# A routed expert loop over 32-token tiles in four column groups, and slot experts in two banks

## The chip, the cores and the metric

One core of a Trainium2 chip runs the whole program. The core has the engines TensorE (PE, with its weight loads PEld), VectorE (DVE), ScalarE (ACT), GpSimd (POOL) and SyncE (SP), and 16 DMA engines. The metric is device time in microseconds (us) of one execution; lower is better. In this program SP issues the plain transfers and POOL the gathers and scatters by row index.

## The reference

Three stages follow one another: a linear attention with decay over 4 x 8 heads, 768 steps and head size 48; a mixture of experts that sends each chosen token to one of 8 experts; and a soft mixture with 8 experts of 4 slots each. All numbers are float32.

```python
N, D, E, F = (3072, 384, 8, 1024)      # tokens, width, experts, hidden width
...
def _moe_ref(x, w_skip, w_gate, w1, w2):
    do_compute = x @ w_skip > 0
    out = x.copy()
    xc = x[do_compute]
    logits = xc @ w_gate
    e_idx = np.argmax(logits, axis=1)
    ...
    for e in range(E):
        mask = e_idx == e
        h = np.maximum(xc[mask] @ w1[e], 0.0)
        y[mask] = gate_w[mask, None] * (h @ w2[e])
    out[do_compute] = xc + y
...
def _moe2_ref(x, phi, w1, w2):
    logits = x @ phi                    # 32 slots, 4 of each expert
    ...
    slot_input = d.T @ x                # d: softmax of logits over the tokens
    for e in range(E):
        slot_out[e] = np.maximum(slot_input[e] @ w1[e], 0.0) @ w2[e]
    return c @ slot_out                 # c: softmax of logits over the slots
```

With these inputs 1514 of the 3072 tokens are sent to an expert: 194, 234, 156, 201, 198, 219, 156 and 156 to the eight.

## The kernel before

The program is one block with an instruction stream written by hand for each engine; semaphores order them, and nothing is reordered by a scheduler. Attention runs over 16 pairs of heads, then the gate, then a sort: DVE and PE work out a list of row numbers (`take_i`, `put_i`) in which each expert's tokens stand together, padded to whole tiles of 128 rows. Two tiles for each of the eight experts make 16 tiles. `tiles_i` holds where each expert's tiles end; every engine loads these numbers into registers and loops to them.

**The routed expert loop.** For a tile, POOL gathers 128 rows from `tokens` in DRAM (L1206), DVE turns them in 16 blocks (L1100, `V.transpose` of 32x96 each), ACT copies the turned rows into `x_t` (L859). PE computes the hidden layer with the weights stationary, 24 products of 128x128 with 128 tokens (L611); ACT applies the ReLU on the way to `h_t` (L856); PE multiplies by `w2` with `h_t` stationary, 8 products of 128x384 (L622). DVE copies the 128x384 result to `ys` (L1105), and POOL scatters it to `results` in DRAM (L1211). A float32 product shows as two PE records. The next tile's rows are gathered and turned while PE works. The weights of expert e + 2 go into the places of expert e (`w1_sb[e % 2]`, `w2_sb[e % 2]`): SP issues both loads when the last result of expert e has landed in DRAM (`load_ffn`, behind `results_stored`), and one matrix of the slot experts behind them.

**Back and slot scores.** SP loads all result rows (L409), DVE adds them to the tokens (L1125), PE turns the new rows (L649) and multiplies them by `phi` (L638). PE runs `idle_products(32)` (L572) while it waits for the rows.

**The slot experts.** Eight experts times two matrices of 1.5 MB. Those of experts 0 to 3 are loaded in the routed loop. The rest wait for places: `e1` of expert 5 goes where the first eight back tiles lay, `e1` of 4 where the next eight lay, and SP issues 4, 5 and 6 together when all 24 back tiles have been added (`x2_ready`). `e1` of 7 and `e2` of 4 and 5 lie in `x_sb` and wait until PE has used it (`slot_parts_full`). PE computes the hidden layers of all eight experts into one PSUM bank (L707, 32 stationary columns, four column groups side by side by `tile_position`, 256 moving columns); then ACT applies one ReLU (L905), PE turns the result (L718), ACT copies it out (L908, L909), and PE runs the eight second layers (L728, four column groups, 384 moving columns).

**Out.** Two small products fold the parts, and PE, ACT, DVE and SP write the 24 output tiles (L745, L920, L1170, L426).

## Time and profile before

| what | us |
|---|---|
| median of 3 runs (433.33 to 436.28) | 434.66 |
| the profiled execution, whole | 430.86 |
| its span on the core | 429.1 |
| PE busy in the span | 390.1 (91%) |
| DVE, ACT, POOL busy | 262.4, 161.9, 103.4 |
| granted PE clock, mean over the span | 0.981 |

The span runs from the first to the last instruction of the core; the whole execution has 1.76 us around it. The profiled execution is 3.8 us faster than the median of the three timed ones. Busy time of PE counts modelled ends of pipelined products, so the time of a stage is read from start to start, not from busy time.

### The profile page before, as it was taken

The page shows a single profiled execution, that of the slowest core. Times are in us where ns is not written, and L with a number is a line of the kernel's source. Part 1 is how long each engine was busy: PE and PEld are TensorE (multiplying, and loading weights), DVE is VectorE, ACT ScalarE, POOL GpSimd, SP SyncE. Part 2 cuts the span into 40 slices and gives each one's busy share as a digit, 9 for nine tenths or more (in the row PEclk, how much of TensorE's full clock was granted, in tenths as well). Part 3 has the DMA queues.
Part 4 walks back from the last instruction along what each step waited for, and adds up shares of the span by engine and source line. Part 5 has one row for each costly group of instructions (what it writes and reads, how often), then busy time and mean ns, then how long its engine had stood idle before and what let it go on. Part 6 is the DMA issues. An engine that isn't in the chain of part 4 may idle for free.

```text
span 429.1 us, 10101 instructions
## 1 busy us (share of the span) xinstructions
PE 390.1 (91%) x3912; PEld 305.5 (71%) x3913; DVE 262.4 (61%) x547; ACT 161.9 (38%) x464; POOL 103.4 (24%) x133
## 2 busy tenths in 40 slices
PE   0799999999999999899999999999999998999861
PEld 0578877777777887777788888888888887855340
DVE  8999999999999346544444444444445354851042
ACT  1567887787678642011111111111111112831031
POOL 2214424443443500312222222222222220020000
PEclk9979999999999999999999999999999998999997
DMA  8957556756779994111485958586767737599929
GB/s 319 388 183 281 217 198 245 249 191 217 256 237 350 397 409 194 38 37 38 171 330 194 324 203 316 216 299 234 279 244 269 259 108 251 215 392 390 373 98 361
DMA packets 40977, 106.97 MB, mean 249 GB/s; under 512 B 3552, under 2 KB 23264, under 8 KB 40432
## 3 DMA queue, kind: packets, MB, share of 16 engines
q1 hardware_dynamic: 38704, 99.62, 62.9%
q0 software_dynamic: 2240, 6.88, 4.7%
q8 instruction: 24, 0.39, 0.4%
q14 instruction: 9, 0.07, 0.1%
HBM read 88.80 MB, written 17.69 MB: 248 GB/s over the span
## 4 chain that ended last, share of the span: by engine, by line
PE 51%; DMA 9%; DVE 6%; issue 1%; ACT 1%; DVEq 0%; POOLq 0%; POOL 0%; ACTq 0%
PE a_bank L611 20%; PE y_bank L622 19%; DMA e_sb<-in_moe_w 4%; DMA x_sb<-in_moe_w 3%; PE a_bank L649 3%; PE a_bank L532 2%; DVE x_sb L1170 1%; PE y_bank L638 1%; DMA results<-ys,put_now 1%; DMA work<-tokens,take_i 1%; DMA back<-results 1%; PE a_bank L669 1%; DVE k_in L955 1%; PE sums_bank L540 1%; ACT bonus_v L790 1%
## 5 line engine op out<-in xcount | busy, mean ns | idle before, releaser
L611 PEld LDWEIGHTS a_bank<-batch_t,w_sb 128*128 128x128 f32 x768 | 88.2, 192 | 5.3 <-issue 1.3
L611 PE MATMUL a_bank<-batch_t,w_sb 128*128 128x128 f32 x768 | 88.4, 275 | 1.1 <-issue 1.1
L1100 DVE STREAM_TRANSPOSE work<-parts 32x96 f32<-32x96 f32 x256 | 69.1, 270 | 28.0 <-DMA parts<-tokens,take_now 24.7
L622 PE MATMUL y_bank<-w_sb,work 128*128 128x384 f32 x256 | 85.2, 486 | 0.0
L1193 POOL TENSOR_SCALAR_AFFINE_SELECT a_sb<-a_sb 128x512 f32<-128x512 f32 x48 | 50.7, 1058 | 86.5 <-ACT a_sb L780 86.5
L622 PEld LDWEIGHTS y_bank<-w_sb,work 128*128 128x128 f32 x256 | 47.4, 190 | 29.7
L856 ACT ACTIVATE work<-a_bank 128x512 f32<-128x512 f32 x32 | 19.1, 597 | 130.8 <-PE a_bank L611 130.8
L1105 DVE COPY ys<-y_bank 128x384 f32<-128x384 f32 x16 | 8.9, 558 | 68.2 <-PE y_bank L622 68.2
L790 ACT ACTIVATE bonus_v<-v_sb,bonus 128x48 f32<-128x48 f32 x192 | 44.9, 327 | 0.0
L469 PE MATMUL a_bank<-r_in,k_in 64*128 64x128 f32 x384 | 36.9, 314 | 1.5 <-DVE r_in L956 0.5
L469 PEld LDWEIGHTS a_bank<-r_in,k_in 64*128 64x128 f32 x384 | 27.2, 200 | 11.7 <-issue 6.7
L933 DVE TENSOR_TENSOR_SCAN decay<-wrk_sb,ones_at 128x780 f32<-128x780 f32 x16 | 28.5, 1778 | 1.2
L942 DVE TENSOR_TENSOR_SCAN decay<-wrk_sb,inv_at 128x780 f32<-128x780 f32 x16 | 28.8, 1802 | 0.1
L780 ACT ACTIVATE a_sb<-a_bank 128x512 f32<-128x512 f32 x48 | 28.5, 593 | 0.6 <-PE a_bank L469 0.6
L490 PE MATMUL y_bank<-r_in,state 64*48 64x128 f32 x320 | 21.4, 276 | 3.9 <-DVE x_sb L969 3.9
L495 PE MATMUL y_bank<-a_sb,v_sb 128*48 128x128 f32 x384 | 24.3, 276 | 0.0
L490 PEld LDWEIGHTS y_bank<-r_in,state 64*48 64x48 f32 x320 | 18.2, 160 | 6.5 <-issue 6.1
L439 PE MATMUL ktok_bank<-ident,k_in 128*128 128x128 f32 x64 | 10.6, 290 | 12.8 <-DVE k_in L955 12.8
L495 PEld LDWEIGHTS y_bank<-a_sb,v_sb 128*48 128x48 f32 x384 | 20.2, 123 | 2.4
L1206 POOL DMA_INDIRECT parts<-tokens,take_now x17 | 18.1, 1064 | 14.6 <-POOL take_now L1236 13.8
L1211 POOL DMA_INDIRECT results<-ys,put_now x17 | 17.8, 1045 | 15.3 <-POOL put_now L1240 14.4
L955 DVE TENSOR_TENSOR k_in<-wrk_sb,decay 128x768 f32<-128x768 f32 x16 | 20.0, 1252 | 0.2 <-PE a_bank L469 0.2
(234 smaller groups left out, 480.9 us busy)
## 6 DMA issues: line engine op xcount, KB each, us to landing
w_sb<-in_moe_w SPq DMA_DIRECT2D x20, 1536.0 KB, 10.7
wrk_sb<-in_wrk SPq DMA_DIRECT2D x16, 768.0 KB, 7.3
e_sb<-in_moe_w SPq DMA_DIRECT2D x8, 1536.0 KB, 14.8
wrk_sb<-in_wrk SPq DMA_DIRECT2D x15, 780.0 KB
v_sb<-in_vt SPq DMA_DIRECT2D x16, 288.0 KB, 2.8
results<-work SPq DMA_DIRECT2D x1, 4608.0 KB, 15.1
tokens<-x_sb SPq DMA_DIRECT2D x4, 1152.0 KB, 14.1
x_sb<-in_moe_w SPq DMA_DIRECT2D x3, 1536.0 KB, 15.4
```

The costliest lines, as they stand in the source:

```text
L469: last = nc.tensor.matmul(a_bank[:, 2 * (g % 2) + a, (c % 2) * C:(c % 2 + 1) * C], k_in[rows, cols], r_in[n % 3][rows, cols], start=True, ...
L490: nc.tensor.matmul(y_cols[64 * a:64 * a + D, c * C:(c + 1) * C], state[n % 2][rows, :, c - 1], r_in[n % 3][rows, c * C:(c + 1) * C], start ...
L495: last = nc.tensor.matmul(y_cols[64 * a:64 * a + D, c * C:(c + 1) * C], v_sb[n % 4][:, c, a, :], a_sb[n % 2][:, a, c, :], start=False, sto ...
L611: last = nc.tensor.matmul(bank[2 + f // 4][:, (f % 4) * P:(f % 4 + 1) * P], w1_sb[j][:, kk, f * P:(f + 1) * P], x_t[:, kk, :], start=(kk = ...
L622: last = nc.tensor.matmul(bank[4][:, 0:DM], h_t[:, f, :], w2_sb[j][:, f, :], start=(f == 0), stop=(f == FK - 1))
L780: nc.scalar.activation(a_sb[n % 2][:, :, 2 * s:2 * s + 2, :].rearrange("p a c t -> p a (c t)"), a_bank[:, 2 * (g % 2):2 * (g % 2) + 2, 0:2 ...
L790: last = nc.scalar.activation(bonus_v[n % 2][:, c, a, :], v_sb[n % 4][:, c, a, :], ACT.Copy, scale=bonus[:, c, a:a + 1])
L933: V.tensor_tensor_scan(decay[:, 0:SCAN], wrk_sb[i][:, 0:SCAN], ones_at[:, :], 0.0, ALU.mult, ALU.add).then_inc(mid_up_ready, 1)
L942: V.tensor_tensor_scan(decay[:, SCAN:2 * SCAN], wrk_sb[i][:, SCAN:2 * SCAN], inv_at[:, :], 0.0, ALU.mult, ALU.add).then_inc(mid_down_ready, 1)
L955: V.tensor_tensor(by_half(k_in[:, :]), by_half(k), half_rows(decay, 0, 3 * NC, True), ALU.mult).then_inc(k_ready, 1)
L1100: last = V.transpose(turned_rows[SQ * o:SQ * (o + 1), :, SQ * i:SQ * (i + 1)], rows_by_block[SQ * i:SQ * (i + 1), :, SQ * o:SQ * (o + 1)])
L1193: nc.gpsimd.affine_select(out=x, in_=x, compare_op=ALU.is_gt, fill=0.0, base=0, pattern=[[0, 2], [0, 2], [1, C]], channel_multiplier=-1).t ...
```

## The change

The routed loop goes over tiles of 32 tokens. Each expert's rows are padded to a multiple of 32 (at least one tile), all of them together to a multiple of 128; the counts above give 7, 8, 5, 7, 7, 7, 5 and 5 tiles, 51, and 52 with the last padding: 13 groups of four. Rows are still gathered and scattered 128 at a time, once for a group.

For a tile the tokens are now stationary (128x32) and the weights move: the hidden layer is 3 x 4 products of 256 columns (`first_layer`), the second 4 x 4 products of 192 columns (`second_layer`), four column groups side by side. PE issues the first layer of a tile before the second layer of the tile ahead of it. DVE turns a group's rows in one instruction (128x384) and the hidden layer in one (128x256); ACT and DVE copy two 32x96 blocks each for a tile's `x_t`; ACT copies two halves of the second layer's result (64x192 each) and DVE adds them in two instructions of 32x192. POOL copies the first 96 rows of a finished group from `ys` to `ys_out`, DVE adds the last 32 there directly. `w2` is laid out in DRAM by partition. SP loads `w1` of expert e + 2 when the last first layer of expert e is done, and `w2` when its last second layer is done. PE runs 42 idle products at the end of the loop in place of 32, and two between the loads of each of the eight loop ends.

`e1` of slot experts 5 and 4 is issued after 8 and 16 added tiles, `e1` of 7 after the first half of the dispatch. The slot experts' hidden layers 0 to 3 and 4 to 7 go to two banks, with a ReLU and a turn for each; the second layers of 0 to 3 start before the second half has been turned.

```diff
...
+            FB = F // PER
+            YW = DM // 2
...
             for e in range(E):
                 j = e % 2
-                over = sp.snap(16 * end + 16)
-                sp.wait_ge(results_stored, over)
-                sp.wait_ge(ld_ffn[j], 32 * (e // 2 + 1))
+                sp.wait_ge(h_full, end)
+                sp.wait_ge(ld_w1[j], 16 * (e // 2 + 1))
                 if e < E - 2:
-                    load_ffn(sp, e + 2)
+                    load_w1(sp, e + 2)
+                sp.wait_ge(ffn_done, end)
+                sp.wait_ge(ld_w2[j], 16 * (e // 2 + 1))
+                if e < E - 2:
+                    load_w2(sp, e + 2)
                     (load_e1, load_e2)[e % 2](sp, e // 2)
...
+            def first_layer(j, x, out):
+
+                for kk in range(DK):
+                    for g in range(PER):
+                        last = nc.tensor.matmul(out[SUB * g:SUB * (g + 1), 0:FB], x[:, kk, :], w1_sb[j][:, kk, FB * g:FB * (g + 1)],
+                                                start=(kk == 0), stop=(kk == DK - 1), tile_position=(0, SUB * g), skip_group_check=True)
+                last.then_inc(h_full, 1)
+
+            def second_layer(j):
+
+                for b in range(FK // 2):
+                    for g in range(PER):
+                        k, d = FK // 2 * (g // 2) + b, YW * (g % 2)
+                        last = nc.tensor.matmul(bank[4][SUB * g:SUB * (g + 1), 0:YW], h_t[:, SUB * k:SUB * (k + 1)], w2_sb[j][:, k, d:d + YW],
+                                                start=(b == 0), stop=(b == FK // 2 - 1), tile_position=(0, SUB * g), skip_group_check=True)
+                last.then_inc(ffn_done, 1)
...
+                with pe.If(first + 1 < end):
+                    with pe.Fori(first + 1, end) as t:
+                        pe.wait_ge(xt_ready_act, t + 1)
+                        pe.wait_ge(xt_ready_dve, t + 1)
+                        pe.wait_ge(h_ready, t)
+                        first_layer(j, x_t, bank[2])
+                        pe.wait_ge(ht_ready, t)
+                        pe.wait_ge(y_parts_ready, t)
+                        second_layer(j)
...
+            def take_x(s, x=x_t):
+
+                for o in range(PER // 2):
+                    last = nc.scalar.activation(x[SUB * o:SUB * (o + 1), :, :],
+                                                turned[SUB * s:SUB * (s + 1), :].rearrange("p (k o t) -> p k o t", o=PER, t=SUB)[:, :, o, :],
+                                                ACT.Copy)
+                last.then_inc(xt_ready_act, 1)
...
+            with act.Fori(0, groups) as g:
+                for s in range(PER):
+                    act.wait_ge(h_full, PER * g + s + 2)
+                    if s == PER - 2:
+                        act.wait_ge(rows_turned, g + 2)
+                    take_x((s + 2) % PER)
+                    act.wait_ge(ht_ready, PER * g + s + 1)
+                    relu_hidden(bank[2], h_ready)
+                    act.wait_ge(ffn_done, PER * g + s + 1)
+                    act.wait_ge(ys_added, PER * g + s + 1)
+                    nc.scalar.activation(y_low, bank[4][0:2 * SUB, 0:YW], ACT.Copy)
+                    nc.scalar.activation(y_high, bank[4][2 * SUB:, 0:YW], ACT.Copy).then_inc(y_parts_ready, 1)
...
+            with dve.Fori(0, groups) as g:
+                for s in range(PER):
+                    dve.wait_ge(h_full, PER * g + s + 2)
...
+                    take_x((s + 2) % PER)
+                    if s == PER - 3:
+                        dve.wait_ge(xt_ready_act, PER * g + s + 3)
+                        dve.wait_ge(xt_ready_dve, PER * g + s + 3)
+                        dve.wait_ge(ld_rows_in, 16 * g + 32)
+                        turn_rows()
+                    dve.wait_ge(h_ready, PER * g + s + 2)
+                    dve.wait_ge(ffn_done, PER * g + s + 1)
+                    turn_hidden()
+                    dve.wait_ge(y_parts_ready, PER * g + s + 2)
...
+                    for d in range(2):
+                        rows = slice(SUB * d, SUB * (d + 1))
+                        last = V.tensor_tensor(place_of[SUB * s:SUB * (s + 1), YW * d:YW * (d + 1)], y_low[rows, :], y_high[rows, :], ALU.add)
+                    last.then_inc(ys_added, 1)
...
+                wait(rows_turned, g + 2)
+                nc.gpsimd.tensor_copy(take_now[:, :], put_i[:, bass.ds(g + 2, 1)]).then_inc(index_ready, 1)
+                wait(index_ready, 2 * g + 3)
+                take_rows()
+                wait(results_stored, 16 * g + 16)
+                nc.gpsimd.tensor_copy(put_now[:, :], put_i[:, bass.ds(g, 1)]).then_inc(index_ready, 1)
+                wait(ys_added, PER * g + PER)
+                nc.gpsimd.tensor_copy(ys_out[0:TOK - SUB, :], ys[0:TOK - SUB, :]).then_inc(ys_taken, 1)
...
```

PE in the routed loop, one expert before (`w_sb` is `w1_sb` or `w2_sb`, `batch_t` holds `x_t`, `work` holds `h_t`):

```order
L606 COMPARE_AND_BRANCH [waits ld_ffn0]
L607 UNCONDITIONAL_BRANCH
L607 ISA
L611 MATMUL a_bank<-batch_t,w_sb 128x128 [waits xt_ready]
L611 MATMUL a_bank<-batch_t,w_sb 128x128 x23
L618 ISA
L622 MATMUL y_bank<-w_sb,work 128x384 [waits ys_full,h_ready]
L622 MATMUL y_bank<-w_sb,work 128x384 x3
L621 REGISTER_ALU
L622 MATMUL y_bank<-w_sb,work 128x384 [waits h_ready]
```

The same place on PE now, for the first expert: the loop, and behind it the first tile of the next expert:

```order
L645 COMPARE_AND_BRANCH [waits ld_w2_0]
L646 UNCONDITIONAL_BRANCH
L646 ISA
L624 MATMUL a_bank<-w_sb,batch_t 32x256 [waits h_ready,xt_ready_dve,xt_ready_act]
L624 MATMUL a_bank<-w_sb,batch_t 32x256 x11
L633 MATMUL y_bank<-w_sb,work 32x192 [waits y_parts_ready,ht_ready]
L633 MATMUL y_bank<-w_sb,work 32x192 x15
L646 REGISTER_ALU
L646 COMPARE_AND_BRANCH
L645 UNCONDITIONAL_BRANCH
L656 REGISTER_ALU [waits ld_w1_1]
L624 MATMUL a_bank<-w_sb,batch_t 32x256 [waits h_ready,xt_ready_dve,xt_ready_act]
```

A pass of the loop is 28 products for 32 tokens where it was 32 products for 128, with a wait ahead of each layer. SP's queue behind the routed loop before (`back` and `w_sb` take the back rows, then weights of the slot experts):

```order
L409 DMA w_sb<-results 128x768 x8
L344 DMA w_sb<-in_moe_w 128x3x1024 [waits x2_ready]
L344 DMA back<-in_moe_w 128x3x1024
L344 DMA w_sb<-in_moe_w 128x3x1024
L344 DMA x_sb<-in_moe_w 128x3x1024 [waits slot_parts_full]
L347 DMA x_sb<-in_moe_w 128x8x384 x2
L347 DMA e_sb<-in_moe_w 128x8x384 [waits slot_hidden_full] x2
```

And now:

```order
L431 DMA w_sb<-results 128x768 x8
L359 DMA back<-in_moe_w 128x3x1024 [waits x2_ready]
L359 DMA w_sb<-in_moe_w 128x3x1024 [waits x2_ready] x2
L359 DMA x_sb<-in_moe_w 128x3x1024 [waits slot_parts_full]
L362 DMA x_sb<-in_moe_w 128x8x384 [waits slot_parts_full]
L362 DMA x_sb<-in_moe_w 128x8x384
L362 DMA e_sb<-in_moe_w 128x8x384 [waits slot_hidden_full] x2
```

The loads are the same; three of them have a wait of their own, and `back` stands first. PE in the slot experts now, from the sixth hidden layer to the second of the second layers (before, the turns L718 and the first L728 stood behind all eight hidden layers):

```order
L749 MATMUL y_bank<-back,batch_t 32x256 x11
L757 MATMUL a_bank<-ident,hid 128x128 [waits slot_hidden_ready]
L757 MATMUL a_bank<-ident,hid 128x128
L703 MATMUL ktok_bank<-ident,comb 128x128 [waits exps_ready]
L703 MATMUL ktok_bank<-ident,comb 128x128 x3
L749 MATMUL y_bank<-w_sb,batch_t 32x256 [waits ld_e1_6]
L749 MATMUL y_bank<-w_sb,batch_t 32x256 x11
L749 MATMUL y_bank<-x_sb,batch_t 32x256 [waits ld_e1_7]
L749 MATMUL y_bank<-x_sb,batch_t 32x256 x11
L765 MATMUL a_bank<-e_sb,work 32x384 [waits ld_e2_0,slot_hidden_t_ready]
L765 MATMUL a_bank<-e_sb,work 32x384 x7
L757 MATMUL a_bank<-ident,hid 128x128 [waits slot_hidden_ready]
```

Both ReLUs now have PE work in front of the turn that needs them.

## Rows read from the trace of the kernel before

**Rows 1.** Busy time in the routed loop: engines with instructions, clock, DMA share, GB/s

```profile
183.00:351.00 168.00, 168.00 (x1024) 134.23 (x1025) 77.15 (x270) 26.79 (x48) 38.43 (x62) 1.00 0.61 224
```

**Rows 2.** Chain that ended last, by time: start, us, what

```profile
181.75 1.14 issue
182.89 5.62 PE a_bank L611 x48
...
193.68 5.36 PE a_bank L611 x48
...
346.31 5.18 PE y_bank L622 x16
351.51 0.57 DVE ys L1105
...
353.39 3.23 DMA results<-ys,put_now
356.64 3.15 DMA back<-results
...
381.89 11.60 DMA x_sb<-in_moe_w
393.80 16.21 DMA e_sb<-in_moe_w
410.05 1.54 PE a_bank L728 x16
```

**Rows 3.** Timeline of PE, column-group products: start, us, then the instruction

```profile
365.38 0.86 PE L638 MATMUL y_bank<-batch_t,phi_sb 128*32 128x128 f32 x24
366.18 1.53 PE L649 MATMUL a_bank<-ident,x_sb 128*128 128x128 f32 x12
...
390.38 1.48 PE L707 MATMUL y_bank<-back,batch_t 128*32 128x256 f32 x24
391.68 1.48 PE L707 MATMUL y_bank<-w_sb,batch_t 128*32 128x256 f32 x24
393.53 1.50 PE L707 MATMUL y_bank<-x_sb,batch_t 128*32 128x256 f32 x24 [0.38 <-DMA x_sb<-in_moe_w]
...
395.54 0.44 PE L718 MATMUL a_bank<-ident,hid 128*128 128x128 f32 x2
...
396.40 4.08 PE L728 MATMUL a_bank<-e_sb,work 128*32 128x384 f32 x48 [0.20 <-ACT work L908]
400.29 1.47 PE L728 MATMUL a_bank<-w_sb,work 128*32 128x384 f32 x16
```

**Rows 4.** Timeline of ACT in the slot experts

```profile
383.58 0.25 ACT L900 ACTIVATE batch_t<-a_bank 128x96 f32<-128x96 f32 x1 [0.26 <-PE a_bank L694]
...
395.10 0.38 ACT L905 ACTIVATE hid<-y_bank 128x256 f32<-128x256 f32 x1 [8.31 <-PE y_bank L707]
396.01 0.33 ACT L908 ACTIVATE work<-a_bank 128x192 f32<-128x192 f32 x1 [0.53 <-PE a_bank L718]
```

**Rows 5.** Groups of DVE and ACT: busy us, mean ns, idle before

```profile
L1100 DVE STREAM_TRANSPOSE work<-parts 32x96 f32<-32x96 f32 x256 | 69.1, 270 | 28.0 <-DMA parts<-tokens,take_now 24.7
...
L1105 DVE COPY ys<-y_bank 128x384 f32<-128x384 f32 x16 | 8.9, 558 | 68.2 <-PE y_bank L622 68.2
L790 ACT ACTIVATE bonus_v<-v_sb,bonus 128x48 f32<-128x48 f32 x192 | 44.9, 327 | 0.0
...
L1063 DVE TENSOR_TENSOR place<-base,place 128x192 f32<-128x192 f32 x1 | 0.4, 357 | 0.0
```

**Rows 6.** Transfers behind the back rows, columns as in Rows 1

```profile
370.00:372.00 2.00, 2.00 (x36) 1.77 (x35) 1.97 (x6) 1.67 (x5) 0.00 (x0) 1.00 0.16 57
372.00:374.00 2.00, 2.00 (x36) 1.66 (x35) 2.00 (x5) 1.84 (x7) 0.00 (x0) 1.00 0.00 0
374.00:376.00 2.00, 1.98 (x48) 1.57 (x50) 0.04 (x1) 2.00 (x6) 0.00 (x0) 1.00 0.17 39
376.00:378.00 2.00, 1.96 (x36) 0.82 (x25) 0.79 (x4) 0.94 (x4) 1.44 (x2) 1.00 1.00 406
```

**Rows 7.** POOL's gathers in the loop (L1206)

```profile
DMA to landing us min/median/max: 3.1/3.2/6.6
```

More of the change, by code:

```diff
@@ L405, in _ @@
                     load_e2(sp, 3)
+            sp.wait_ge(results_stored, over)
             for q in range(NT // 2):
@@ L579, in _ @@
             nc.tensor.matmul(a_bank[:, 1, 0:E * NT], not_before[:, :], flat, start=True, stop=True).then_inc(rank_full, 1)
-            def sorted_transposes():
-                for kk in range(DK):
-                    last = nc.tensor.transpose(bank[0][:, kk * TOK:(kk + 1) * TOK], xs[:, kk * P:(kk + 1) * P],
-                                               ident[:, :])
-                last.then_inc(xs_used, 1)
             idle_products(20)
@@ new lines, in _ @@
+            pe.wait_ge(ld_w1[0], 16)
+            pe.wait_ge(xt_ready_act, 1)
+            pe.wait_ge(xt_ready_dve, 1)
+            first_layer(0, x_first, bank[0])
+            for e in range(E):
+                j = e % 2
+                first, end = ends[e], ends[e + 1]
+                pe.wait_ge(ld_w2[j], 16 * (e // 2 + 1))
+                with pe.If(first + 1 < end):
[7 more added lines that the diff above has]
+                        second_layer(j)
+                if e < E - 1:
+                    pe.wait_ge(ld_w1[1 - j], 16 * ((e + 1) // 2 + 1))
+                    pe.wait_ge(xt_ready_act, end + 1)
+                    pe.wait_ge(xt_ready_dve, end + 1)
+                    pe.wait_ge(h_ready, end)
+                    first_layer(1 - j, x_t, bank[2])
+                else:
+                    pe.wait_ge(xt_ready_act, end + 1)
+                    pe.wait_ge(xt_ready_dve, end + 1)
+                    pe.wait_ge(h_ready, end)
+                    nc.tensor.matmul(bank[3][:, 0:P], ident[:, :], ident[:, :], start=True, stop=True).then_inc(h_full, 1)
+                pe.wait_ge(ht_ready, end)
+                pe.wait_ge(y_parts_ready, end)
+                second_layer(j)
@@ L631, in slot_scores @@
+            pe.wait_ge(h_ready, ends[E] + 1)
+            idle_products(42)
             def slot_scores(q):
@@ L701, in _, with slot_hidden @@
             N = F // groups
-            for e in range(E):
+            def slot_hidden(e):
                 pe.wait_ge(ld_e1[e], 16)
@@ L732, in _ @@
                 last.then_inc(slot_back_done, 1)
+            exps = comb[:, :, :].rearrange("p (q i) s -> p q (i s)", i=BATCH)
+            for e in range(EH + 2):
+                slot_hidden(e)
+            pe.wait_ge(slot_hidden_ready, 1)
+            turn_slot_hidden()
+            pe.wait_ge(exps_ready, 1)
+            turn(exps, comb_transposed, 0, 4, bank[6])
+            for e in range(EH + 2, E):
+                slot_hidden(e)
+            pe.wait_ge(slot_hidden_t_ready, 1)
+            slot_back(0)
+            pe.wait_ge(slot_hidden_ready, 2)
+            turn_slot_hidden()
+            for e in range(1, EH):
+                slot_back(e)
+            turn(exps, comb_transposed, 4, NB, bank[7])
+            pe.wait_ge(slot_hidden_t_late, 1)
+            for e in range(EH, E):
+                slot_back(e)
             pe.wait_ge(parts_ready, 2)
@@ new lines, in _ @@
+            act.wait_ge(routed, 1)
+            groups = act.value_load(tiles_i[0:1, E + 1:E + 2], min_val=0, max_val=MAX_GROUPS)
+            act.wait_ge(rows_turned, 1)
+            take_x(0, x_first)
+            take_x(1)
+            act.wait_ge(h_full, 1)
+            relu_hidden(bank[0], h_first)
+            with act.Fori(0, groups) as g:
[10 more added lines that the diff above has]
+                    nc.scalar.activation(y_high, bank[4][2 * SUB:, 0:YW], ACT.Copy).then_inc(y_parts_ready, 1)
@@ L863, in copy_logits @@
+            done = act.snap(PER * groups + 2)
+            act.wait_ge(xt_ready_act, done)
+            act.wait_ge(h_ready, PER * groups + 1)
+            act.wait_ge(y_parts_ready, PER * groups + 1)
             def copy_logits(q):
@@ L1107, in _, with turn_rows, take_x, turn_hidden @@
-            fetched = dve.snap(16 * total + 16)
+            def turn_rows():
+                V.transpose(turned, rows_in).then_inc(rows_turned, 1)
+            def take_x(s, x=x_t):
+                for o in range(PER // 2, PER):
+                    last = V.tensor_copy(x[SUB * o:SUB * (o + 1), :, :],
+                                         turned[SUB * s:SUB * (s + 1), :].rearrange("p (k o t) -> p k o t", o=PER, t=SUB)[:, :, o, :])
+                last.then_inc(xt_ready_dve, 1)
+            def turn_hidden():
+                V.transpose(h_t, hid[:, :]).then_inc(ht_ready, 1)
@@ L1108, in _ @@
+            fetched = dve.snap(16 * groups + 32)
             dve.wait_ge(ld_rows_in, fetched)
@@ L1277, in pack, with by_quarters @@
     return wrk, vt, ublock.reshape(P, -1)
+def by_quarters(w):
+    import numpy as np
+    E, F, DM = w.shape
+    return np.ascontiguousarray(w.reshape(E, 4, F // 128, 32, DM).transpose(0, 1, 3, 2, 4).reshape(E, 128, -1))
 def kernel(**inputs):
```

239 lines of the change are left out of this document (114 added, 125 removed).

## The prediction

> **What bounds the kernel now.** I read the chain of waits in order of time first. From 182.89 to 346.31 + 5.18 = 351.49 it stays on PE and alternates between two rows, 5.36 us for a tile's hidden layer (L611) and 5.16 to 5.18 for its second layer (L622) [rows 2]. The reader is to see that nothing else stands between them: 351.49 - 182.89 = 168.60 us for 16 tiles is 10.54 each, which is 5.36 + 5.18. So loop returns, changes of expert, gathers and weight loads cost PE nothing here. The busy times of the same stretch agree: PE 168.00 of 168.00 at full clock, DVE 77.15, ACT 26.79, DMA share 0.61 [rows 1]. What makes PE's time smaller in this stage shortens the program, until another engine is late.
>
> The second place is the slot experts. PE starts them at 383.58 + 0.25 + 0.06 = 383.89 (ACT's L900 ends, PE follows) and ends them at 410.05 + 1.54 = 411.59 [rows 4, 2]: 27.70 us. Here the chain goes over transfers: 11.60 us and then 16.21 us of weights [rows 2]. The windows show why they are late: the queue is almost empty for some 5.3 us (0.32 us busy in 370 to 372, none in 372 to 374, 0.34 in 374 to 376), and full from 376 on [rows 6]. SP waits there for all 24 added tiles.
>
> **The routed loop, PE.** The new first layer has the shape of the slot experts' hidden layer: 12 products, 24 records, 32 stationary columns, 256 moving, four column groups. One such group of 24 takes 391.68 - 390.38 = 1.30 us, 54 ns a record [rows 3]. The second layer is 32 records of 192 columns, a shape the trace lacks. Records of 384 columns take (400.29 - 396.40) / 48 = 81 ns, of 128 columns (366.18 - 365.38) / 24 = 33 ns [rows 3]. Half of 81 is 40.5, a line between 33 and 54 gives 44. I take 41, since from 256 to 384 the cost goes by columns: 32 x 41 = 1.31 us. The ends are 33 ns (1.06 us) and 54 ns (1.74 us). A tile of 32 is then 2.61 us, and the reference's token counts give 52 of them: 135.7 us in place of 168.60, **-32.9**. A tile of 128 costs about the same as four of 32 (10.4); the gain is padding, 1664 rows in place of 2048.
>
> **The routed loop, the other engines.** PE pays these times only if nobody makes it wait. PE issues first layer t + 1, then second layer t. Between two first layers it has a second layer of 1.31 us to do, and in that time ACT must copy the next tokens and apply the ReLU, since `x_t` and bank 2 exist once. That chain: from the end of PE's issue to ACT 395.10 - (393.53 + 1.30) = 0.27, two copies of 96 columns at 0.25, ReLU of 256 columns 0.38, ACT to PE 395.54 - (395.10 + 0.38) = 0.06 [rows 3, 4]: 1.21 us, 0.10 less than the cover. Between two second layers stands a first layer of 1.30: ACT needs 0.27 + 2 x 0.33 + 0.06 = 0.99 for the two halves [rows 4], DVE 0.27 + 0.45 + 0.06 = 0.78 for the turned hidden layer (0.45 by a line between 270 ns for 96 columns and 558 for 384 [rows 5]). Behind the halves DVE adds (2 x 0.36 [rows 5]) until 1.70 after the second layer's issue, copies tokens (2 x 0.27) until 2.30 with the handover, and is awaited at 2.61. Sums for a tile: ACT 1.54, DVE 0.54 + 0.45 + 0.72 + a quarter of 0.56 = 1.85. All below 2.61, so I take no wait; the margin of 0.10 is the thinnest of the whole account.
>
> POOL's gather for the next group but one starts when a group is turned and has a group's time, 10.4 us; the longest landing of before is 6.6 [rows 7], with some 2 us of index work ahead of it. POOL's copy of 96 rows is awaited two tiles later. Neither is on the path. **Weights:** an expert's w1, w2 and one slot matrix are 4.7 MB, 11.6 us at the 406 GB/s of a full queue [rows 6]; the shortest expert lasts 5 x 2.61 = 13.1. SP now waits on PE's own counts, some microseconds earlier than the landed result. Cost nothing; if the queue gave only the loop's mean of 224 GB/s [rows 1], the 3.1 MB that PE needs would take 14 us and the two short experts with loads behind them would wait about 1 to 2 us each, so 0 to 4.
>
> **Entry, expert changes, exit.** At the entry PE spends 1.14 us on issue alone: two loads of loop ends, a branch and two loop heads [rows 2]. Now the eight ends are loaded while the gather runs. By that row eight loads take at most 4.6 us; the gather's landing of 3.2, DVE's turn of 0.56 and the copies of 0.54 are 4.3. I take **-1.1**, with +0.3 as the other end. The eight changes of expert could cost up to 1.14 each, 9.1 in all; I take 0, the value that the 16 tiles in eight loops show. At the exit, the time from the last product to the first back row read was 356.64 - 351.49 = 5.15. The two halves and the add are 0.27 + 0.66 + 0.06 + 0.72 = 1.71 where one copy was 0.57 + 0.02; against it POOL's index copy, which made most of 353.39 - 352.08 = 1.31 between copy and scatter, is done ahead [rows 2]. **0**, from -0.2 to +1.1. Ten more idle products of PE cover a wait; they cost only if the rows come sooner than they end, under 1 us.
>
> **Slot experts.** PE's own work is 16 groups at 1.30, 20.8 us; the stretch between the last hidden layer's issue (394.83) and the first second layer (396.40) has 1.57 us of turns and waits, to which one more turn of 0.44 comes [rows 3]: 22.8 us, end at 406.7. The transfers: the first two matrices are queued behind the back rows, so the 5.3 us gap closes, and the last group ends at 411.59 - 5.3 = 406.3. PE is then the later one by a little: 411.59 - 406.7 gives **-4.9**. The ends are 0 (the gap opens elsewhere) and -5.3.
>
> **Sum:** -32.9 - 1.1 + 0 - 4.9 = -38.9. The profiled execution of 430.86 would become 392.0; it lies 3.8 below the median of the runs, and I take the difference from the median: 434.66 - 38.9 = **395.8**.
>
> **Rivals.** (A) *The copies set the pace.* ACT's 0.25 is from one row that reads PSUM; copies of 48 columns from SBUF take 0.327 with a scale [rows 5]. With 0.33 for a copy and a handover of 0.27 in both directions the chain is 0.27 + 0.66 + 0.38 + 0.27 = 1.58, 0.27 more than its cover: 52 x 0.27 = 14, **410**. Against it speak the 0.06 of ACT to PE and ACT's low sum. The Trainium skill ("TensorEngine Tiling (Array Packing)", Performance Considerations) says that tiling speeds up TensorE but not the emptying of PSUM, and that after a fourfold speed-up the copies may become the bottleneck. By that rule this rival decides; ACT's 26.79 us in 168 show no sign of it, but no row here has the small tiles. Chance 0.22, spread over 402 to 418.
>
> (B) *Slower: the loop's return costs.* PE's loop body now runs 2.61 us and returns 36 times (52 tiles in eight loops, one first tile of each outside), where it returned eight times. If the chip had to fetch the body anew at each return, the shortest transfer of 3.1 us [rows 7] is the nearest row for it: 36 x 3.1 = 112, near **507**. It turns the gain into a loss from 38.9 / 36 = 1.1 us for a return. Against it: a return of before costs nothing [rows 2]. The Trainium skill ("Runtime: NRT & Kernel Launch", Instruction fetch mechanics) says that a taken branch to a target outside the two pages at hand makes the engine fetch before it goes on. The old loop, of similar length, shows no such stall, so the trace speaks against it here. Chance 0.03.
>
> (C) *The second layer doesn't go by columns.* At 54 ns a record it is 1.74 us: 52 x 0.43 = 22, **418**, chance 0.05; at 33 ns 52 x 0.25 = 13 less, **383**, chance 0.04, if then ACT's chain were not the bound, which it nearly is.
>
> (D) *The slot experts gain nothing*, since the early matrices only move the gap: 395.8 + 4.9 = **400.7**, chance 0.06.
>
> **How the numbers follow.** The forecast has 0.60: 389 to 402, by the smaller bounds (weights +4, exit +1.1, a part of the expert changes above; a second layer a few ns a record cheaper below) and the runs' spread of 1.6. With D and the part of A up to 411 (0.14) this is 0.80, so the range is **389 to 411**. What a measurement of this kernel can tell from no change is about 1%, 4.3 us. All cases but B are faster by more than that: 0.96; B gives 0.03 slower; 0.01 is left for gains and losses that cancel.
>
> **What would show it.** The new profile should have first layers 2.61 us apart on PE with no idle rows in the loop, at full clock; 24 records in 1.30, 32 in 1.31; the loop from about 181.8 to 317.5. Under A, PE idles ahead of the first layers behind ACT's ReLU, by 0.1 to 0.5 us each. Under B, it idles by issue at the loop's line. In the slot experts the windows should have no empty stretch behind the back rows, and the second layers of experts 4 to 7 should follow without a wait for weights. The forecast is wrong if PE's idle time in the loop is over 8 us, or if a transfer ends a wait in it.

## The result and the profile after

The changed kernel takes 398.9 us (median of 4 runs, 398.3 to 400.5), the kernel before 434.17 (4 runs beside it, 433.33 to 436.28): ratio 0.9187, 95% interval 0.9142 to 0.9231. The profiled execution of after has a span of 396.7 us and took 398.49; that of before had 429.1 and 430.86. PE's granted clock averages 0.981 in both.

By stage, from the chain of waits and the timeline of the two profiled executions:

| stage | before, us | after, us | difference | predicted |
|---|---|---|---|---|
| start of the loop's first product | 182.89 | 181.65 | -1.2 | -1.1 |
| routed loop | 168.60 | 141.87 | -26.7 | -32.9 |
| back rows and slot scores, to the slot experts' first product | 32.40 | 32.77 | +0.4 | 0 |
| slot experts | 27.70 | 22.88 | -4.8 | -4.9 |
| output | 17.51 | 17.53 | 0.0 | 0 |

The loop of after is taken to end at 322.22 + 1.30 = 323.52; the modelled end of its last product, 0.24 later, falls into the next line. The rows sum to -32.4, which is the difference of the spans (429.1 to 396.7). The medians differ by 35.3: the profiled execution of before lay 3.3 below its median, that of after 0.4 below.

The chain of waits of after, in order of time (start, length, what), where [rows 2] had two rows of over 5 us in turn:

```profile
181.72 2.73 PE a_bank L624 x48
184.44 1.30 PE y_bank L633 x32
185.74 1.39 PE a_bank L624 x24
187.14 1.30 PE y_bank L633 x32
188.44 1.38 PE a_bank L624 x24
189.82 1.30 PE y_bank L633 x32
191.12 1.47 PE a_bank L624 x24
...
319.76 1.63 PE y_bank L633 x32
...
322.22 1.54 PE y_bank L633 x32
...
324.93 0.36 DVE work L1226
...
326.18 2.66 DMA results<-work,put_now
...
329.72 5.18 DMA back<-results
...
356.29 7.98 PE y_bank L749 x144
...
373.83 5.34 PE a_bank L765 x64
```

The second layers (L633) are 1.30 us, 41 ns a record, as forecast, but for six of 1.39 to 1.43 with a first layer of 1.29 or 1.30 behind each. The first layers (L624) are otherwise not 1.30 but 1.38 and 1.39, and 1.47 once in four tiles, when ACT also waits for a newly turned group. The last second layer has no first layer beside it: it starts at 322.22, 2.67 after the one ahead of it (319.55 in the timeline; a piece of the chain starts only where the modelled end of the group ahead lies) in place of 1.30, and waits for the halves (L937) in between. From 329.72 on the chain is the old one, and in the slot experts no DMA stands in it any more.

What holds the first layers is seen in the timeline (start, length, engine, instruction, and the idle time ahead with its releaser), one tile inside the loop:

```profile
208.39 1.35 PEld L633 LDWEIGHTS y_bank<-w_sb,work 128*32 128x32 f32 x32
208.61 1.51 PE L633 MATMUL y_bank<-w_sb,work 128*32 128x192 f32 x32
208.87 0.57 ACT L911 ACTIVATE batch_t<-work 32x96 f32<-32x96 f32 x2 [0.72 <-PE a_bank L624]
...
209.47 0.38 ACT L917 ACTIVATE hid<-a_bank 128x256 f32<-128x256 f32 x1
...
209.97 1.05 PEld L624 LDWEIGHTS a_bank<-w_sb,batch_t 128*32 128x32 f32 x24 [0.23 <-issue]
210.00 1.50 PE L624 MATMUL a_bank<-w_sb,batch_t 128*32 128x256 f32 x24
```

From the second layer's first product, ACT starts its two copies after 208.87 - 208.61 = 0.26, ends them and the ReLU at 209.85, and PE's first product comes at 210.00, 0.15 later: 1.39 us, where PE was ready after 1.30. PE itself looks busy all the time (1.51 of modelled length against 1.39 to the next start), so the page of after shows the loss only as idle time of the weight loads (columns as in [rows 5]):

```profile
L633 PE MATMUL y_bank<-w_sb,work 128*32 128x192 f32 x1664 | 78.5, 326 | 0.7 <-ACT work L937 0.7
L624 PE MATMUL a_bank<-w_sb,batch_t 128*32 128x256 f32 x1248 | 77.9, 381 | 0.0
...
L624 PEld LDWEIGHTS a_bank<-w_sb,batch_t 128*32 128x32 f32 x1248 | 42.2, 109 | 24.7 <-issue 11.0
L911 ACT ACTIVATE batch_t<-work 32x96 f32<-32x96 f32 x108 | 30.4, 281 | 45.3 <-PE a_bank L624 32.1
```

A copy takes 281 ns, not 250. In the tile of 1.47 (first layer at 212.76) the turn of the new group ended at 210.30, 1.3 us before ACT's copies, so it isn't DVE that is late there; ACT starts its copies 0.34 and not 0.26 behind the second layer, with one wait more ahead of them. The windows of after over the stage where the queue was empty in [rows 6], columns as there:

```profile
332.00:344.00 12.00, 11.31 (x141) 8.98 (x140) 11.28 (x23) 8.21 (x21) 0.00 (x0) 1.00 1.02 391
344.00:356.00 12.00, 11.83 (x160) 7.30 (x158) 5.43 (x18) 6.90 (x21) 0.79 (x2) 1.00 1.02 403
```

The gap of 5.3 us is gone: the queue is full at 391 to 403 GB/s.

### The profile page after: what moved, and what is told of

Read it like the earlier page. It is cut to its first block, busy times and chain, and to the rows that moved or that the text cites. A ratio compares the mean times of both kernels' runs of the same rounds, so it can differ in the third digit from the quotient of the medians.

```text
span 396.7 us, 14472 instructions
## 1 busy us (share of the span) xinstructions
PE 364.4 (92%) x5811; PEld 278.1 (70%) x5811; DVE 276.1 (70%) x557; ACT 219.6 (55%) x682; POOL 103.6 (26%) x136
## 4 chain that ended last, share of the span: by engine, by line
PE 55%; DVE 6%; DMA 2%; issue 1%; ACT 1%; SPq 0%; DVEq 0%; ACTq 0%; POOLq 0%
PE a_bank L624 18%; PE y_bank L633 17%; PE y_bank L749 3%; PE a_bank L765 3%; PE a_bank L557 2%; PE a_bank L690 2%; DVE x_sb L1292 1%; PE a_bank L597 1%; DMA back<-results 1%; PE y_bank L679 1%; PE y_bank L520 1%; PE a_bank L710 1%; DMA results<-work,put_now 1%; DVE k_in L1041 1%; PE y_bank L515 1%
## 5 line engine op out<-in xcount | busy, mean ns | idle before, releaser
L633 PE MATMUL y_bank<-w_sb,work 128*32 128x192 f32 x1664 | 78.5, 326 | 0.7 <-ACT work L937 0.7
L624 PE MATMUL a_bank<-w_sb,batch_t 128*32 128x256 f32 x1248 | 77.9, 381 | 0.0
L633 PEld LDWEIGHTS y_bank<-w_sb,work 128*32 128x32 f32 x1664 | 63.6, 110 | 10.8 <-DVE work L1194 3.4
L624 PEld LDWEIGHTS a_bank<-w_sb,batch_t 128*32 128x32 f32 x1248 | 42.2, 109 | 24.7 <-issue 11.0
L911 ACT ACTIVATE batch_t<-work 32x96 f32<-32x96 f32 x108 | 30.4, 281 | 45.3 <-PE a_bank L624 32.1
L1194 DVE STREAM_TRANSPOSE work<-hid 128x256 f32<-128x256 f32 x53 | 23.3, 440 | 35.2 <-PE y_bank L633 32.8
L1226 DVE TENSOR_TENSOR ys<-work 32x192 f32<-32x192 f32 x78 | 27.2, 348 | 8.7 <-ACT work L937 6.6
L936 ACT ACTIVATE work<-y_bank 64x192 f32<-64x192 f32 x52 | 16.8, 324 | 23.2 <-PE y_bank L633 22.9
L1189 DVE COPY batch_t<-work 32x96 f32<-32x96 f32 x108 | 26.4, 245 | 2.7 <-PE a_bank L624 0.4
L515 PEld LDWEIGHTS y_bank<-r_in,state 64*48 64x48 f32 x320 | 18.2, 160 | 6.4 <-issue 5.9
L597 PE MATMUL a_bank<-ident 128*128 128x128 f32 x172 | 22.0, 290 | 0.4 <-DVE take_i L1170 0.3
```

Of the source, the lines that this page charges most:

```text
L515: nc.tensor.matmul(y_cols[64 * a:64 * a + D, c * C:(c + 1) * C], state[n % 2][rows, :, c - 1], r_in[n % 3][rows, c * C:(c + 1) * C], start ...
L624: last = nc.tensor.matmul(out[SUB * g:SUB * (g + 1), 0:FB], x[:, kk, :], w1_sb[j][:, kk, FB * g:FB * (g + 1)], start=(kk == 0), stop=(kk = ...
L633: last = nc.tensor.matmul(bank[4][SUB * g:SUB * (g + 1), 0:YW], h_t[:, SUB * k:SUB * (k + 1)], w2_sb[j][:, k, d:d + YW], start=(b == 0), s ...
L911: last = nc.scalar.activation(x[SUB * o:SUB * (o + 1), :, :], turned[SUB * s:SUB * (s + 1), :].rearrange("p (k o t) -> p k o t", o=PER, t= ...
L1226: last = V.tensor_tensor(place_of[SUB * s:SUB * (s + 1), YW * d:YW * (d + 1)], y_low[rows, :], y_high[rows, :], ALU.add)
```

## The experiments

Theory 1, formed on these rows: the loop is bound by ACT's chain of copies, ReLU and two handovers, some 0.1 us a tile above PE's cover; the loop's gain is padding; the slot experts' gain is the earlier transfers and not the two banks. The rivals, by part: DVE, POOL or the loop's return sets the pace; small tiles are cheaper or dearer by themselves; two banks make the gain.

**Fewer copies on ACT, and more.** ACT copies one of the four 32x96 blocks of a tile's tokens and DVE three; in the second kernel the other way round. The edit of the first, ACT's lines and then DVE's:

```diff
-                for o in range(PER // 2):
+                for o in range(1):
...
-                for o in range(PER // 2, PER):
+                for o in range(1, PER):
```

> ACT copies one of a tile's four 32x96 blocks and DVE three, where each copied two; nothing else is changed. In the new profile a first layer starts 1.38 us behind the second layer ahead of it, 0.09 later than that layer lasts. Theory 1 (ACT's chain of copies, ReLU and handover, 0.26 + 0.60 + 0.38 + 0.14, is longer than its cover): the chain becomes 1.09, first layers stand 1.30 behind, about 4.5 us of the loop go, and up to 1 more at the group changes: 393.5 to 395. Theory 2 (the 0.09 is PE's own return and wait handling, as the label issue says): no change, 398.9. A third, that DVE then becomes late with the turned hidden layer in one tile of four: part of the gain goes, 395 to 398.

394.51 us, ratio to before 0.9115 (0.9076 to 0.9154). Its timeline at one tile:

```profile
234.25 1.51 PE L633 MATMUL y_bank<-w_sb,work 128*32 128x192 f32 x32
234.52 0.28 ACT L911 ACTIVATE batch_t<-work 32x96 f32<-32x96 f32 x1 [0.67 <-PE a_bank L624]
234.62 0.76 DVE L1189 COPY batch_t<-work 32x96 f32<-32x96 f32 x3
234.83 0.38 ACT L917 ACTIVATE hid<-a_bank 128x256 f32<-128x256 f32 x1
235.55 1.50 PE L624 MATMUL a_bank<-w_sb,batch_t 128*32 128x256 f32 x24
```

ACT is done at 235.21, a copy earlier, and the first layer follows 1.30 after the second: PE's own pace. First layers now follow after 1.30 to 1.37 (one after 1.70); the loop is 137.6 us instead of 141.9.

> The other way round: ACT copies three of a tile's four blocks and DVE one. Theory 1 (ACT's chain is awaited already, so every nanosecond more is paid): the chain grows by one copy of 0.30, about 50 first layers come 0.30 later, 15 us, near 414. Rival (the chain had slack and the gap was PE's own): the first 0.1 to 0.2 of it is covered, 5 to 10 us, 404 to 409.

413.89 us, 0.9581 (0.9526 to 0.9637). One copy more on ACT costs 15.0 us, 52 x 0.29. Together the two say that ACT's copies are the bound at two a tile: a copy more is paid in full, a copy less gives back nearly all that PE's cover leaves. DVE isn't the bound: it has a copy less in the second kernel, and that one is slower.

**Padding alone.** The rows of an expert are padded to 128 again, in the new loop: 64 tiles of 32 where the change has 52.

```diff
-            link(V.tensor_scalar(n_rows[:, :], cum[:, :, NT - 1], (SUB - 1) / 2.0, SUB_ROUND, ALU.add, ALU.add))
-            link(V.tensor_scalar(n_rows[:, :], n_rows[:, :], SUB_ROUND, float(SUB), ALU.subtract, ALU.max))
+            link(V.tensor_scalar(n_rows[:, :], cum[:, :, NT - 1], (TOK - 1) / 2.0, ROUND, ALU.add, ALU.add))
+            link(V.tensor_scalar(n_rows[:, :], n_rows[:, :], ROUND, float(TOK), ALU.subtract, ALU.max))
```

> Each expert's rows are padded to 128 again in the new kernel, so that the loop has 64 tiles of 32 in place of 52. Theory 1 (the gain of the loop is padding alone): 12 tiles at 2.69 us more, 32 us, near 431, and the kernel keeps only the gain of the slot experts over the kernel before. Rival (column groups or the shorter pipeline give a part): the 12 tiles cost the same, but then the whole must stay clearly below the old 434 by more than the slot experts' 4.8, under 425.

432.0 us, 0.9986 (0.9951 to 1.0021). Twelve tiles cost 428.8 - 396.7 = 32.1 us of span, 2.68 each. With the old padding the small tiles gain nothing in the loop: it takes 174 us, from 181.1 to 355.1, against 168.6 before, since four tiles take 10.82 us in this trace and one of 128 tokens took 10.54 [rows 2]; the 4.8 of the slot experts makes good for that.

**Slot experts: transfers or banks.** First the early loads undone with two banks kept, then one bank with the early loads kept, then the early loads alone in the kernel before.

```diff
-            sp.wait_ge(x2_ready, RING)
+            sp.wait_ge(x2_ready, NT)
+            load_e1(sp, 4)
             load_e1(sp, 5)
-            sp.wait_ge(x2_ready, 2 * RING)
-            load_e1(sp, 4)
-            sp.wait_ge(x2_ready, NT)
             load_e1(sp, 6)
-            sp.wait_ge(slot_parts_full, 1)
+            sp.wait_ge(slot_parts_full, 2)
             load_e1(sp, 7)
-            sp.wait_ge(slot_parts_full, 2)
```

> The slot experts' matrices e1 of 5, 4 and 7 are issued as late as in the kernel before; the two banks stay. Theory 1 (the earlier transfers carry the slot experts' gain): the queue is empty again for some 5 us behind the back rows, the last second layers wait for weights, 3.5 to 5 us slower, 402.5 to 404. Rival (PE's own 22.9 us bind and the transfers have slack): under 1 us slower.

404.83 us, 0.9361 (0.9312 to 0.9409), 5.9 above after, somewhat more than expected. Its windows and its timeline of PE:

```profile
332.00:344.00 12.00, 11.42 (x143) 9.09 (x142) 11.46 (x24) 8.32 (x21) 0.00 (x0) 1.00 0.90 339
344.00:346.00 2.00, 2.00 (x36) 1.60 (x35) 2.00 (x5) 1.81 (x5) 0.00 (x0) 1.00 0.00 0
```

```profile
378.05 1.50 PE L762 MATMUL a_bank<-e_sb,batch_t 128*32 128x384 f32 x16 [1.62 <-DMA e_sb<-in_moe_w]
382.19 2.79 PE L762 MATMUL a_bank<-e_sb,batch_t 128*32 128x384 f32 x16 [2.65 <-DMA e_sb<-in_moe_w]
```

The empty queue is back, and the last two second layers wait for their weights. The stage takes 28.85 us, 1.15 more than the 27.70 of before, with two banks. That excess, and the miss, is the clock: the last group runs at a granted clock of 0.50 (window 382.1 to 385.1) and takes 2.79 us, where the last one of before ran at 1.00 and took 1.50.

```diff
-                        last = nc.tensor.matmul(bank[4 + e // EH][NS * g:NS * (g + 1), 0:N], slot_m[:, e, kk, :],
...
+                        last = nc.tensor.matmul(bank[4][NS * g:NS * (g + 1), 0:N], slot_m[:, e, kk, :],
...
-            for e in range(EH + 2):
+            for e in range(E):
...
             pe.wait_ge(slot_hidden_t_ready, 1)
-            slot_back(0)
-            pe.wait_ge(slot_hidden_ready, 2)
...
+                if e == 6:
+                    pe.wait_ge(slot_hidden_t_late, 1)
```

> The slot experts' hidden layers go to one bank with one ReLU and one turn behind all eight, as in the kernel before; the early transfers stay. Theory 1 (PE is bound by its own work, and the split saves only the wait of about 0.9 us for the ReLU and its copy and costs a turn of 0.4): 0 to 1 us slower, 399 to 400. Rival (the two banks carry the gain of the stage): 3 to 5 us slower, 402 to 404.

397.58 us, 0.9193 (0.9153 to 0.9232). The stage in its chain of waits:

```profile
355.07 10.57 PE y_bank L749 x192
...
367.12 10.69 PE a_bank L765 x128
```

It is 22.74 us against 22.88: the second bank is worth nothing here. The whole is 1.3 us below after, where 0 to 1 above was expected, but most of that lies ahead of the stage: in the profiles the loop starts 0.7 earlier and is 0.35 shorter.

> The kernel before with one part of the change alone: SP issues e1 of the slot experts 5, 4 and 7 early; one bank, the loop of 128-token tiles. Theory 1 (the earlier transfers are the whole gain of that stage, and independent of the loop): 4 to 5.5 us faster than before, ratio 0.987 to 0.991. Rival (the stage needs the two banks too, or the gain was a shift from the loop): ratio 0.996 to 1.000.

425.93 us, 0.9856 (0.981 to 0.9901), with one bank and the old loop: 6.6 us below the 432.54 of before in the same series, a little more than expected. The stage has no transfer in its chain any more:

```profile
383.60 10.57 PE y_bank L710 x192
...
395.53 10.57 PE a_bank L731 x128
```

It is 22.5 us, 5.2 less than before. So the transfers carry the whole gain of the slot experts, and it doesn't depend on the loop.

**Weight loads.** SP waits for four tiles more before it loads an expert's next weights.

```diff
+                later = sp.snap(end + 4)
-                sp.wait_ge(h_full, end)
+                sp.wait_ge(h_full, later if e < E - 1 else end)
...
-                sp.wait_ge(ffn_done, end)
+                sp.wait_ge(ffn_done, later if e < E - 1 else end)
```

> SP issues the next weights four tiles later (some 10.7 us) than in the new kernel, about when the old rule, a landed result, would have let it. Theory 1 (transfers have no slack worth 10.7 us, since the short experts last 13.4 us and w1 and w2 take about 8 of a full queue and 2 more to land): PE waits for weights behind the three five-tile experts and a little at others, 8 to 18 us slower, 407 to 417. Rival (the queue has slack enough): under 2 us.

420.71 us, 0.9739 (0.9682 to 0.9796): +21.8, more than expected. PE in its timeline:

```profile
237.07 1.50 PE L625 MATMUL a_bank<-w_sb,batch_t 128*32 128x256 f32 x24 [2.72 <-DMA w_sb<-in_moe_w]
...
243.46 2.79 PE L625 MATMUL a_bank<-w_sb,batch_t 128*32 128x256 f32 x24 [3.58 <-DMA w_sb<-in_moe_w]
...
316.83 1.78 PE L625 MATMUL a_bank<-w_sb,batch_t 128*32 128x256 f32 x24 [2.73 <-DMA w_sb<-in_moe_w]
318.32 2.86 PE L634 MATMUL y_bank<-w_sb,work 128*32 128x192 f32 x32
...
325.54 2.81 PE L634 MATMUL y_bank<-w_sb,work 128*32 128x192 f32 x32
```

Five such waits make 13.0 us. Behind three of them PE is slower: the first layers take 2.79, 1.78 and 1.97 us in place of 1.50, and the second layers behind those 1.62, 2.86 and 2.81 in place of 1.51, 4.8 more. The windows show the clock behind the first two waits (the eighth column is the granted clock):

```profile
237.00:239.00 2.00, 1.93 (x40) 1.59 (x44) 0.35 (x2) 0.36 (x2) 0.00 (x0) 1.00 0.87 332
243.40:246.30 2.90, 2.85 (x30) 1.59 (x34) 0.00 (x1) 0.00 (x1) 0.00 (x0) 0.51 0.88 324
```

In the second layers of 318.32 and 325.54 it is 0.50. Together that is nearly all of the 18.2 us by which the loop is longer. Of the 2.3 that are left of the difference of the spans (417.2 to 396.7), 2.1 are the last scatter, which takes 4.73 us to land (344.28) in place of 2.66. After itself has no such wait: early weights are needed there, and they come in time.

**The exit and POOL's copy.**

```diff
-            idle_products(42)
+            idle_products(32)
```

> The new kernel with 32 idle products at the end of the loop, as before. In the new profile 42 end at 333.1, 0.4 us after the first added row, and PE's clock stays full; before, PE was idle and its clock at half there. Theory 1 (DVE's 24 adds of 0.55 set the pace of that stage): within 0.5 us, 398.4 to 399.4. Rival (the clock at half costs PE time that ends up on the path): 1.5 to 2.5 us slower.

399.58 us, 0.9243 (0.9203 to 0.9283), span 396.8 against 396.7: the ten more idle products cost and gain nothing that shows. What a halved clock would cost there stays open, since it didn't halve: PE is idle for 1.64 us ahead of the first turned rows and its granted clock stays 1.00; before, it was idle for 1.87 us (to 360.49) and the clock was 0.50 from 362 to 365.

In the next kernel DVE copies the 96 finished rows in place of POOL.

```diff
+                        dve.wait_ge(ys_added, PER * g + PER)
+                        V.tensor_copy(ys_out[0:TOK - SUB, :], ys[0:TOK - SUB, :]).then_inc(ys_taken, 1)
...
-                wait(ys_added, PER * g + PER)
-                nc.gpsimd.tensor_copy(ys_out[0:TOK - SUB, :], ys[0:TOK - SUB, :]).then_inc(ys_taken, 1)
```

> DVE, not POOL, copies the first 96 rows of a finished group from ys to ys_out, once for each of the 13 groups, ahead of its last add there. Theory 1 (DVE has slack in the loop: it is idle for some 0.6 us ahead of each turned hidden layer; POOL's copy only keeps it off a queue that isn't the bound): the copy of some 0.3 to 0.5 us is absorbed but for the first copies of tokens behind it, 0 to 4 us slower, 399 to 403. Rival (POOL's copy shares DVE's path to memory and slows it): faster by 1 us or more.

401.27 us, 0.9274 (0.9237 to 0.9311), 2.4 above after. A tile takes 2.747 us there and 2.706 in after. That DVE's copy costs this is likely, but not shown: this run also had the late signals of the next paragraph.

**The two that seemed better, together.** The copies of the first experiment joined to the single bank:

> The two edits that cost nothing or gained, together: DVE copies three blocks and ACT one, and the slot experts use one bank. Theory 1 (the loop's gain of 4.4 us is ACT's chain and independent of the slot experts, where one bank and two cost the same within 0.2): 393.5 to 394.7. Rival (the 1.3 us by which one bank was quicker is real and comes on top): 392.5 to 393.4.

402.57 us, 0.9303 (0.9266 to 0.934): 8 us slower than with the copies alone, although the single bank works behind the loop and cost nothing by itself. The stage of the slot experts is 22.6, as it should be; the loss is in the loop. Its timeline:

```profile
234.60 1.51 PE L633 MATMUL y_bank<-w_sb,work 128*32 128x192 f32 x32
...
235.94 1.50 PE L624 MATMUL a_bank<-w_sb,batch_t 128*32 128x256 f32 x24
236.72 0.32 ACT L930 ACTIVATE work<-y_bank 64x192 f32<-64x192 f32 x1 [1.09 <-PE y_bank L633]
236.80 0.45 DVE L1185 STREAM_TRANSPOSE work<-hid 128x256 f32<-128x256 f32 x1 [0.95 <-PE y_bank L633]
...
237.42 0.74 DVE L1217 TENSOR_TENSOR ys<-work 32x192 f32<-32x192 f32 x2 [0.18 <-ACT work L931]
...
237.53 1.51 PE L633 MATMUL y_bank<-w_sb,work 128*32 128x192 f32 x32
...
238.19 0.76 DVE L1180 COPY batch_t<-work 32x96 f32<-32x96 f32 x3
...
239.05 1.50 PE L624 MATMUL a_bank<-w_sb,batch_t 128*32 128x256 f32 x24
```

ACT and DVE both wait for the second layer of 234.60 and both start over 2.1 us after it, where 1.57 is usual; PE runs its next layer meanwhile as if nothing were amiss. The trace's semaphore updates say the same: that of a second layer's last product (`ffn_done`) comes 360 ns after that product's start in most tiles, in this run 830 to 928 in every fourth tile and 547 to 582 in another. DVE then turns the hidden layer late, so the second layer of 237.53 comes 0.3 late (1.59 after the first layer, 1.30 is PE's pace), and DVE's adds and three copies behind that hold up the first layer of 239.05 by 0.2 more. Four tiles take 11.15 us on the mean, and 10.48 with the copies alone: 13 x 0.67 = 8.7 us, as the loops say (146.3 against 137.6).

Late signals were then found in the first profile of after too (614 to 879 ns in 19 of 52 tiles) and in the runs with three copies on ACT, late weights, fewer idle products and DVE's row copy. The four of the experiments above that were run together first (three copies on DVE, padding, the early loads undone, one bank) had none. To learn whether the late signals belong to the build, two kernels were run again beside each other:

> The same edit as in the first experiment (DVE copies three of four row blocks), run again in one job with the changed kernel. In the run that joined this edit to the single bank, the second layer's completion signal came 901 ns after the start of its last product in every fourth tile and 550 ns in another, where it is 360 ns in the other tiles; the same edit alone had 360 ns in all 52 tiles, and so had every kernel of the one job it was run in, while the kernels of the other jobs had late signals. Theory A: the lateness belongs to the place of the run and not to the build. Then this kernel and the changed kernel both show 360 ns in all tiles (and 394.5 beside 397 to 398 us), or both show late signals in one or two tiles of four; in that case this kernel loses its lead, since its first layer has no slack left, and comes to 400 to 402.5 beside 399. Theory B: the lateness belongs to the build. Then this kernel shows 360 ns in all tiles and 394.5 us wherever it runs, and the changed kernel shows 620 to 850 ns in some.

> The changed kernel as it is, beside the run above on the same chip. Theory A (place): its completion signals are all at 360 ns if those of the run above are, with a median of 397 to 398 us; else it shows late ones as in its first profile, at 398.5 to 400 us. Theory B (build): late signals of 620 to 850 ns in three tiles of eight as in its first profile and 398.5 to 400 us, while the run above has none and stands 4 to 5 us below.

With three copies on DVE 395.17 us (394.86 to 396.25), ratio to before 0.9125 (0.906 to 0.919); after 398.91 (398.13 to 398.96), 0.9198 (0.9133 to 0.9263). Neither has one late signal: all 52 are within 360 to 370 ns. So theory B falls: the same build of after had 19 in one run and none in another. All kernels with the new loop that were run together were alike (none in two of the four series, late ones in two, and in after's first run), which is what theory A asks; but a chip of the same number had had late signals in one of those series, some 13 minutes earlier, so the place alone hardly is the cause. What causes them stays open. After loses next to nothing by them: 2.706 us a tile with them, 2.705 without, and 0.3 us ahead of the last second layer; its median without them is 398.9 again, a little over the 397 to 398 expected. The joined kernel, whose single bank stands behind the loop, loses some 9 us in the run that had them. It was run once: what it takes without them, and whether the kernel with three copies on DVE would lose as much with them, was not tried.

## Why the prediction was right, and where it was off

*Bound and sum.* PE did set the pace of the loop before, and the shorter work on PE is what the program gained. The sum said -38.9, the profiled executions -32.4, the medians -35.3. The error of 6.5 in the traces is nearly all in one term, the loop (-26.7 for -32.9). That the forecast of 395.8 is only 3.1 off is luck for the other half: the sum was read from a profiled execution below the median and taken off the median; off the profiled time it would have been 392.0 against 398.5.

*The loop, PE.* Both layers cost what the rows promised: 24 records 1.30, 32 records 1.30 (41 ns each). Rival C is out in both directions. That the gain is padding was right, and more so than the 10.4 for four tiles against 10.54 said: four take 10.82, and with 2048 rows again the loop is 5.4 us slower than the old one. The padding gives 32.1 us, and the small tiles take 5.4 of them back.

*The loop, the other engines.* This is the term that was mis-sized. The step "1.21 us, 0.10 less than the cover" measured 1.39, 0.09 over it: copies 0.30 apart in place of 0.25 (a row that copied from PSUM stood in for the same size elsewhere), and ACT to PE 0.15 in place of 0.06. That 0.06 came from a stretch of straight code with one wait; here PE waits for three semaphores, some of them against a loop counter, which may be the reason; no run tests it. The 50 pairs of a second and a first layer take 2.706 us on the mean, 0.106 over 2.60: 5.3 us in all, 1.0 of it the 0.08 more in tiles with a newly turned group. The last second layer, which has no first layer beside it, waits 2.67 - 1.30 = 1.4 (0.3 of it a late signal). Together 6.7, and 52 x 2.60 + 6.7 = 141.9, the loop's time; the forecast had 135.7. (DVE's turn by the line that the prediction names is 0.43, not 0.45; it measured 0.45, and DVE wasn't the late one.)

*Rival A* described this mechanism, with 0.27 a tile; it came with a third of that, so the time stayed within the forecast's own case of 389 to 402. Of the signs that the prediction set, first layers 2.61 us apart with no wait failed (2.71); the loop's loss of 6.7 us stayed under the 8 of idle time that it allowed, and no transfer ends a wait of PE there. The Trainium skill ("TensorEngine Tiling (Array Packing)", Performance Considerations) has the rule that copies out of PSUM may become the bound after a fourfold speed-up of TensorE, and that both ScalarE and VectorE should share them. The traces bear it out in part: ACT's chain, with one such step (the ReLU), binds by 0.09 us a tile. But TensorE had no such speed-up here (4 x 2.60 = 10.4 us of products for four tiles against 10.54 for one of 128), and the copies whose move took 3.7 to 4.4 us off read SBUF (`turned`, a part of `work`).

*Rival B.* No return of the loop shows idle time on PE; a tile issued outside the loop follows at the same 2.68 us as one inside.

*Entry, exit, expert changes.* -1.2, +0.4 and nothing that shows, against -1.1, 0 and 0. The agreement at the entry says little: over the traces the new loop starts at 180.9 to 183.1, the old one at 182.9 and, in the kernel with the early transfers alone, at 182.2. POOL's index copy is done ahead as said, but POOL still starts the scatter 0.9 us after the last add.

*Weights.* Cost nothing, as said. That the cover is needed is shown by the late loads: +21.8.

*Slot experts.* -4.8 against -4.9, by the mechanism named first, the gap in the queue. The second bank, which the prediction counted as one more turn of 0.44, neither helps nor hurts (22.74 against 22.88). Rival D is out.

## What to carry to other kernels

When a faster engine hands work to and fro every 2.6 us, write out the whole chain of the next slowest engine with its two handovers, and take the handovers from rows with the same kind of waits; a margin of 0.10 us that rests on a handover of 0.06 is none. Then move a copy to the engine with time to spare: three of four blocks on DVE give 394.5 to 395.2 us, the fastest version here and 0.9% below the changed kernel run beside it, both times without late signals. And ask of every gain by smaller tiles how much of it is padding, since that part hangs on the data alone.

## What the runs showed of the hardware beyond that

The signal that a group of products is done may come late: 360 ns after the last product's start as a rule, but 450 to 1150 ns in some tiles of the loop in five of the profiled experiments and the first run of after, for the most part at the same places of every four or eight tiles, while PE's next products run on time. It hits all who wait for that semaphore at once. The row of PE doesn't show it: it ends 326 ns after the product's start in either case.

The Trainium skill ("Perfetto Trace Analysis", Tensor Engine Instruction (MATMUL, LD_WEIGHTS)) says that a product's end in the profile is computed and that the semaphore is pushed only when PSUM has acknowledged the writes. The traces fit that order, with some 0.03 us from the row's end to the signal, or up to 0.8; no run here shows what holds the acknowledgement.

In the run with late weights TensorE's next group ran at a granted clock of 1.00, the level of 2.4 GHz, behind waits of 1.34 and 2.72 us (1.50 us for the group), and at 0.51, about that of 1.2 GHz, behind 3.58 (2.79 us). Behind 2.73 and 2.68 it fell during the next group (1.78 and 1.97 us), and the second layer after that ran at 0.50 (2.86 and 2.81 in place of 1.51). In the run with the early loads undone it was 0.50 behind 2.65 us. So the length of the wait alone didn't settle it, and a late transfer can cost more than its wait.
